# Attention values with rounded and low parts side by side as one stationary matrix

## The reference

```python
scores = q @ k.T / 8, causal; a = softmax(scores)
local = a @ v
q_p = phi(q)                       # where(x > 0, x, exp(x) - 1) + 1
mem_out = (q_p @ M_prev) / (q_p @ z_prev + 1e-06)
out = g * mem_out + (1 - g) * local     # g = sigmoid(beta), per head
x = out as [2304 tokens, 512]
x = elu(x @ w_in1) @ w_out1
x = (h * clip(h + 3, 0, 6) / 6) @ w_out2, h = x @ w_in2
```

## Time and profile before

| | us |
|---|---|
| median of 3 runs (1120.95 to 1123.28) | 1121.03 |
| the profiled execution | 1122.92 |
| its span | 1121.1 |
| PE busy (share of the span) | 1076.2 (96%) |
| DVE busy | 677.8 (60%) |
| ACT busy | 298.4 (27%) |
| POOL busy | 192.5 (17%) |

### The profile page before, as it was taken

One profiled execution on the slowest core, in us unless ns is written; L12 is line 12 of the kernel. 1 busy time (PEld: TensorE's weight loads), 2 busy tenths in 40 slices (PEclk: granted clock), 3 DMA queues, 4 the chain that ended last, 5 costly groups with the idle time before them and its releaser, 6 DMA issues.

```text
span 1121.1 us, 16386 instructions
## 1 busy us (share of the span) xinstructions
PE 1076.2 (96%) x6080; PEld 966.3 (86%) x6080; DVE 677.8 (60%) x1278; ACT 298.4 (27%) x737; POOL 192.5 (17%) x202
## 2 busy tenths in 40 slices
PE   5999999999889999999999999899999999999998
PEld 2667676676879999999999999898999999899997
DVE  5676766767388544545454468865656565565654
ACT  3666666666432212112121123301001010000100
POOL 3434434344265000000000025500000000000000
PEclk9999999999889999999999999999999999999999
DMA  4322121220134000000000014100000000000000
GB/s 162 119 97 101 52 101 56 98 101 20 38 113 132 1 1 1 0 0 0 0 0 0 0 37 131 57 1 13 15 0 28 0 28 0 0 28 0 28 0 28
DMA packets 16599, 44.56 MB, mean 40 GB/s; under 512 B 1968, under 2 KB 1968, under 8 KB 16560
## 3 DMA queue, kind: packets, MB, share of 16 engines
q1 hardware_dynamic: 16560, 44.05, 11.3%
HBM read 39.33 MB, written 4.72 MB: 39 GB/s over the span
## 4 chain that ended last, share of the span: by engine, by line
PE 89%; DVE 6%; issue 3%; ACT 1%; DMA 1%; SPq 0%; DVEq 0%
PE ps L473 35%; PE ps L494 18%; PE ps L486 17%; PE ps L450 8%; PE ps L384 3%; DVE pt_lo L751 2%; PE ps L379 1%; PE ps L459 1%; PE ps L428 1%; PE ps L418 1%; PE ps L387 1%; DVE x_all L795 1%; ACT r_rows L570 1%; PE ps L405 1%; DVE h_hi L824 1%
## 5 line engine op out<-in xcount | busy, mean ns | idle before, releaser
L473 PE MATMUL ps<-x_hi,w 128*128 128x384 f32 x1536 | 392.5, 336 | 0.0
L473 PEld LDWEIGHTS ps<-x_hi,w 128*128 128x128 f32 x1536 | 280.9, 189 | 7.4
L473 PE MATMUL ps<-x_lo,w 128*128 128x384 f32 x768 | 258.3, 336 | 0.0
L486 PE MATMUL ps<-h_hi,w 128*128 128x384 f32 x768 | 196.6, 336 | 6.0 <-DVE h_lo L826 6.0
L494 PE MATMUL ps<-w,h_hi 128*128 128x512 f32 x576 | 179.2, 392 | 3.1 <-DVE h_lo L826 3.1
L824 DVE CAST h_hi<-act_tmp 128x384 fp32r<-128x384 f32 x192 | 108.9, 567 | 100.9 <-PE ps L486 53.2
L486 PEld LDWEIGHTS ps<-h_hi,w 128*128 128x128 f32 x768 | 139.5, 189 | 7.0 <-DVE h_lo L826 7.0
L473 PEld LDWEIGHTS ps<-x_lo,w 128*128 128x128 f32 x768 | 144.7, 188 | 0.0
L296 POOL TENSOR_TENSOR w<-stage,w 128x1024 f32 (+1 forms) x32 | 77.7, 2436 | 358.3 <-ACT w L544 358.3
L486 PE MATMUL ps<-h_lo,w 128*128 128x384 f32 x384 | 129.0, 336 | 0.0
L494 PEld LDWEIGHTS ps<-w,h_hi 128*128 128x128 f32 x576 | 106.8, 188 | 22.1 <-issue 2.4
(11 more groups left out here) (110 smaller groups left out, 1233.8 us busy)
## 6 DMA issues: line engine op xcount, KB each, us to landing
nat<-nat_in SPq DMA_DIRECT2D x16, 768.0 KB, 5.4
qk<-qk_t SPq DMA_DIRECT2D x16, 608.0 KB, 3.8
stage<-w_in SPq DMA_DIRECT2D x32, 256.0 KB, 2.7
stage<-w_out SPq DMA_DIRECT2D x32, 256.0 KB, 2.9
out<-rows_out SPq DMA_DIRECT2D x18, 256.0 KB, 2.1
beta_sb<-beta SPq DMA_DIRECT2D x1, 4.0 KB, 6.5
```

Source lines behind the costliest of these rows:

```text
L473: mm = pe.matmul(ps[:, bank:bank + CHUNK], w[:, n, wp, 0, cols], xp[:, m, :], start=(m == 0 and part == 0), stop=(m == KM - 1 and part == 2))
L486: mm = pe.matmul(ps[:, Y_AT + 512 * m:Y_AT + 512 * m + CHUNK], w[:, n, wp, 1, cols], hp[:, n % 2, :], start=(n == 0 and part == 0), stop=( ...
```

## The change

V's rounded and low parts of one head stand side by side in one stationary matrix (`v_split`: 64 columns rounded, 64 low), and M's likewise (`m_split`). One pass with the rounded probabilities and one with the low ones replace three; the first 64 output partitions hold the rounded part's products, the other 64 those of the low part. (The product of both low parts is now added too.) Each head has an output bank of its own (banks 6 and 7) for rows 128 to 575. The rows 0 to 127 of both heads come in a piece of their own, `first_rows(p)`, behind `times_m(p)`, into a ring bank: the ring has a new place Q0 between G and C00. M's matmuls for rows 128 on take 64 rows of the array, one head each.

ScalarE's `low_rows(p)` copies the lower 64 partitions to SBUF at the head of slot 1, ahead of C00; VectorE's `sum_x(p)` adds them to the upper 64 in four pieces, in slot 1 behind the maximum and ahead of the row statistics; GpSimd's `store_x(p)` multiplies by the factors, between `phi_by_z(p+2)` and `split_vm(p+2)`.

```diff
+RING = (G, Q0, C00, C01, C10, C11, C2, C3, RMAIN, PHI, TAIL)
 # GpSimd
+            def store_x(p):
+                x = x_all[:, p * S:p * S + S]
+                pool.wait_ge(x_summed, p + 1)
+                pool.wait_ge(q0_summed, p + 1)
+                pool.wait_ge(r_done, p + 1)
+                pool.wait_ge(pt_hi_done, LOS * (p + 1))
+                pool.tensor_tensor(x, x, r_rows[:, :], ALU.mult).then_inc(x_stored, 1)
...
                     phi_by_z(p)
+                if p >= 2:
+                    store_x(p - 2)
+                if p < PAIRS:
                     split_vm(p)
 # TensorE: chunk_free
+                at = RING.index(c) - 2
+                before, q = RING[at], p if at >= 0 else p - 1
+                if before == Q0 and q >= 1:
+                    pe.wait_ge(q0_summed, q)
+                elif before == RMAIN and q >= 0:
+                    pe.wait_ge(r_done, q + 1)
+                elif before != Q0 and q >= 0:
+                    pe.wait_ge(pt_lo_done, LOS * q + LO_RANK[before] + 1)
 # times_v, times_m, first_rows
-                        pe.wait_ge(x_stored, p)
+                        pe.wait_ge(x_summed, p)
+                lo = max(P * t, P)
                 for a in range(2):
-                    for lo, hi in zip(cuts, cuts[1:]):
-                        for part, (v, pt) in enumerate(((v_hi, pt_hi), (v_lo, pt_hi), (v_hi, pt_lo))):
+                    for part, pt in enumerate((pt_hi, pt_lo)):
+                        mm = pe.matmul(ps[:, x_at(a) + lo - P:x_at(a) + S - P], v_tile(u, a, t), blocks(pt, a, t, lo, S),
+                                       start=(t == 0 and part == 0), stop=False)
...
+                for part, ph in enumerate((phi_t_hi, phi_t_lo)):
+                    for a in range(2):
+                        d = slice(D * a, D * a + D)
+                        mm = pe.matmul(ps[:, x_at(a):x_at(a) + S - P], m_tile(u, a)[d], ph[d, P:S], start=False, stop=(part == 1))
...
+            def first_rows(p):
+                u, at = p % 2, ring_at(p + 1, Q0)
+                chunk_free(p + 1, Q0)
+                for a in range(2):
+                    for part, pt in enumerate((pt_hi, pt_lo)):
+                        pe.matmul(ps[:, at + P * a:at + P * a + P], v_tile(u, a, 0), blocks(pt, a, 0, 0, P),
+                                  start=(a == 0 and part == 0), stop=False)
+                for part, ph in enumerate((phi_t_hi, phi_t_lo)):
+                    for a in range(2):
+                        mm = pe.matmul(ps[:, at + P * a:at + P * a + P], m_tile(u, a), ph[:, 0:P], start=False, stop=(a == 1 and part == 1))
+                mm.then_inc(q0_done, 1)
 # ScalarE
+            def low_rows(p):
+                if p >= 1:
+                    act.wait_ge(x_summed, p)
+                    act.wait_ge(q0_summed, p)
+                act.wait_ge(pv_done, 6 * (p + 1))
+                heads = ps[D:P, x_at(0):x_at(0) + 1024].rearrange("p (a q) -> p a q", a=2)
+                act.activation(x_low[D:P, :, P:S], heads[:, :, 0:S - P], ACT.Copy).then_inc(x_low_done, 1)
+                act.wait_ge(q0_done, p + 1)
+                at = ring_at(p + 1, Q0)
+                act.activation(x_low[D:P, :, 0:P], ps[D:P, at:at + 2 * P].rearrange("p (a q) -> p a q", a=2), ACT.Copy).then_inc(x_low_done, 1)
 # VectorE
+            def sum_x(p):
+                at, q0 = p * S, ring_at(p + 1, Q0)
+                dve.wait_ge(x_low_done, 2 * p + 1)
+                for a in range(2):
+                    add = dve.tensor_tensor(x_all[D * a:D * a + D, at + P:at + S], ps[0:D, x_at(a):x_at(a) + S - P], x_low[D:P, a, P:S], ALU.add)
+                add.then_inc(x_summed, 1)
+                dve.wait_ge(x_low_done, 2 * p + 2)
+                for a in range(2):
+                    add = dve.tensor_tensor(x_all[D * a:D * a + D, at:at + P], ps[0:D, q0 + P * a:q0 + P * a + P], x_low[D:P, a, 0:P], ALU.add)
+                add.then_inc(q0_summed, 1)
...
+                    if s == 1 and g >= 2:
+                        sum_x(g - 2)
                     if s == 1 and g >= 1:
                         row_stats(g - 1)
-                    if s == 1 and g >= 2:
-                        store_x(g - 2)
```

More of the change, by code:

```diff
@@ L105, in build @@
     phi = sb("phi", [2, QT, P])
[L106 to L109, removed]
+    v_split = sb("v_split", [2, QT, 2, 2, D], F32R)
+    m_split = sb("m_split", [2, 2, 2, D], F32R)
+    x_low = sb("x_low", [2, S])
     prob = sb("prob", [2, P_ALL])
@@ L150, in ring_at, with x_at @@
     def ring_at(p, c):
-        return 512 * (4 + (CHUNKS_OF * p + c) % 2)
-    X_AT = 7 * 512 - X_CUT
+        return 512 * (4 + (len(RING) * p + RING.index(c)) % 2)
+    def x_at(a):
+        return 512 * (6 + a)
     Y_AT = 4 * 512
@@ L178, in build @@
     pv_done = semaphore("pv_done")
+    q0_done = semaphore("q0_done")
+    x_low_done = semaphore("x_low_done")
+    x_summed = semaphore("x_summed")
+    q0_summed = semaphore("q0_summed")
     x_stored = semaphore("x_stored")
@@ L209, in build, with v_raw, v_tile, m_tile @@
     rows_sent = semaphore("rows_sent")
[L211 to L219, removed]
+    def v_raw(u):
+        return nat[:, u, 0:QT * P].rearrange("p (t a d) -> p t a d", t=QT, a=2)
+    def v_tile(u, a, t):
+        return v_split[:, u, t, a].rearrange("p h d -> p (h d)")
+    def m_tile(u, a):
+        return m_split[:, u, a].rearrange("p h d -> p (h d)")
     def rows_of(buf, i, a):
@@ L305, in split_vm @@
                 pool.wait_ge(nat_loaded[u], 16 * (p // 2 + 1))
-                if p == 0:
-                    pool.wait_ge(zeros_ready, 2)
                 if p >= 2:
[L309 to L312, removed]
+                    pool.wait_ge(q0_done, p - 1)
+                m_raw = nat[:, u, 2 * QT * P + P:NAT].rearrange("p (a d) -> p a d", a=2)
+                pool.tensor_scalar(m_split[:, u, :, 0], m_raw, 1.0, 1.0, ALU.mult, ALU.mult).then_inc(vm_rounded, 1)
+                pool.tensor_copy(v_split[:, u, :, :, 0], v_raw(u)).then_inc(vm_rounded, 1)
                 pool.wait_ge(vm_rounded, 2 * p + 2)
-                pool.tensor_tensor(m_lo[:, u, :], m_raw, m_hi.bitcast(F32)[:, u, :], ALU.subtract)
-                pool.tensor_tensor(v_placed(v_lo, u), v_all(nat, u), v_placed(v_hi.bitcast(F32), u), ALU.subtract).then_inc(vm_split, 1)
+                pool.tensor_tensor(m_split[:, u, :, 1], m_raw, m_split.bitcast(F32)[:, u, :, 0], ALU.subtract)
+                pool.tensor_tensor(v_split[:, u, :, :, 1], v_raw(u), v_split.bitcast(F32)[:, u, :, :, 0], ALU.subtract).then_inc(vm_split, 1)
+            def store_x(p):
[5 more added lines that the diff above has]
+                pool.tensor_tensor(x, x, r_rows[:, :], ALU.mult).then_inc(x_stored, 1)
             def phi_by_z(p):
@@ L358, in _ @@
             for n in range(APART, STAGES):
+                if n == EARLY:
+                    store_x(PAIRS - 1)
                 lo_weights(w[:, n], n, n)
@@ L413, in turn @@
                 elif c in (C2, C3):
-                    t = 2 + c - C2
+                    t = 2 if c == C2 else 3
                     for a in range(2):
@@ L510, in _ @@
                         times_m(g - 2)
+                        first_rows(g - 2)
                     if s == 2 and g >= 1:
@@ L521, in _ @@
             times_m(PAIRS - 1)
+            first_rows(PAIRS - 1)
             for n in range(KF):
@@ L549, in exp_rows @@
                 if s == 0 and p == 0:
-                    act.wait_ge(zeros_ready, 3)
+                    act.wait_ge(zeros_ready, 1)
                 if s == 0 and p >= 2:
@@ L577, in round_chunk @@
                     a, t = (c - C00) % 2, (c - C00) // 2
+                    if p >= 1 and c == C00:
+                        act.wait_ge(q0_done, p)
                     cp = act.activation(blocks(pt_hi, a, t, P * t, EDGE), ps[:, at:at + EDGE - P * t], ACT.Copy)
                 elif c in (C2, C3):
-                    t = 2 + c - C2
+                    t = 2 if c == C2 else 3
                     if c == C3 and p >= 1:
@@ L647, in _ @@
                 for s in range(QT):
+                    if s == 1 and g >= 2:
+                        low_rows(g - 2)
                     if g >= 1:
@@ L658, in _ @@
                         act.wait_ge(small_free, 1)
+                        act.wait_ge(x_stored, PAIRS - B + 1)
                         x_round(0, 0)
@@ L666, in _ @@
                         exp_tile(0, 0)
+            low_rows(PAIRS - 1)
             act.wait_ge(x_stored, PAIRS)
@@ L853, in _ @@
                         x_rest(0, 0)
-            store_x(PAIRS - 1)
+            sum_x(PAIRS - 1)
             for n in range(KF):
```

26 lines of the change are left out of this document (3 added, 23 removed).

## The result

| | before | after |
|---|---|---|
| median of 4 runs (lowest to highest) | 1122.03 us (1120.95 to 1123.28) | 1149.92 us (1148.77 to 1150.75) |
| ratio, 95% interval | | 1.0248 (1.0230 to 1.0265) |
| profiled execution: time, span, mean clock | 1122.92, 1121.1, 0.993 | 1150.63, 1148.4, 0.969 |

The forecast was 1153 us, from 1122 to 1166. The changed kernel is slower by 27.9 us.

A forecast was written before the change was run, and what follows sets the result against it. TensorE, busy 16.37 of 17.50 us per pair, looked like the bound, with relays through VectorE and ScalarE; 9 x 3.3 + 5 x 0.65 - 1.1 = +31.9 us on the 1121.03 median gave 1153 us, range 1122 to 1166.

The forecast's parts named there:

- TensorE ahead of the scores of slot 1, +0.32: TensorE's tile 4, M, first rows and switch back take 2.12 us against 1.80, so slot 1's scores start 0.32 later.
- rival 4: M's 64-row matmuls run one after another, adding 0.4 us ahead of the sums and 6 us to the total.
- The sums, 1.60: VectorE's four sums behind slot 1's maximum take 1.60 us, the middle of 1.44 overlapped and 1.76 end to end.
- C01's wait, idle time 2.7, key tile 0 later by 1.7, factors by 0.15: C01's transposes wait for the last sum: TensorE idle 2.7 us, key tile 0 1.7 later, factors 0.15 later.
- The saving behind it: Shorter TensorE work on key tiles 0 and 1, behind C01's wait, gives back 1.52 us per pair.
- Line 306 beside phi, 0.5: GpSimd's last queued operation moves beside VectorE's phi operations, one of which waits 0 to 0.73 us, taken as 0.5.
- A pair without a fall, +0.65: A steady attention pair at full clock grows by 0.65 us: 0.15 at the factors plus 0.5 at phi.
- Falls, 9 of 14 at +3.3: TensorE's new idle time drops the clock to 1.2 GHz in 9 of 14 pairs, each such pair 3.3 us longer.
- The total, +31.9: Whole kernel: 9 x 3.3 + 5 x 0.65 - 1.1 = +31.9 us, giving a median of 1153 us.
- Rival 1: The clock stays up and pairs cost 0.65 us, from 0.15 to 1.1: +2 to +14, centre 1129 us; chance 0.28.
- Group 1, -1.1: The first group with changed code has no sums before it and gains key tile 0's saving: -1.1 us.

The follow-up runs named there:

- experiment 9: Changed kernel with the four sums ordered by head, 448 and 128 columns of head 0, then of head 1: 1146.09 us in one run.
- experiment 1: Changed kernel with five unused f32 matmuls of 288 columns ahead of C01's transposes in groups 2 to 15, filling TensorE's idle time: 1142.20 us, ratio 1.0189.
- experiment 2: Changed kernel with VectorE summing the first rows before the two 448-column pieces, so C01 waits for the small sums only: 1145.30 us, ratio 1.0214.
- experiment 3: Changed kernel with VectorE's sums moved ahead of the maximum of slot 1: 1125.47 us, ratio 1.0036 to the kernel before.
- experiment 8: Changed kernel with only the row statistics moved ahead of the maximum, the sums still behind it: 1142.17 us, ratio 1.0183.
- experiment 5: Changed kernel with the sums ahead of the maximum and GpSimd's product at the head of its round: 1120.43 us, ratio 0.9991.
- experiment 6: Changed kernel with VectorE's slot 1 in the order row statistics, sums, maximum, low parts: 1108.01 us, ratio 0.9877 to the kernel before.
- experiment 4: Changed kernel with GpSimd's product of x and the factors moved to the head of its round: 1163.41 us, ratio 1.0377.

## Why the prediction held, and what it missed

- **TensorE ahead of the scores of slot 1, +0.32.** The scores of slot 1 begin 2.60 us after chunk G, before it was 2.19: +0.41. M's four 64-row matmuls take 0.60 (161.21 to 161.81) against 0.68 taken; rival 4 is out.
- **The sums, 1.60.** They take 1.89 (165.49 to 167.38), above the end-to-end bound of 1.76, since each takes a little more than taken and none overlaps the next. The middle was the wrong choice: the output changes its half of the partitions three times within the four, and experiment 9 shows that each change keeps an operation from overlapping the one before. The Trainium skill, page "VectorE: DVE Perf Modes", section "Two Vector instructions with no wait between them", had said so, and the trace agrees: by its rule the four sums came to 1.76, 0.16 above the term taken and nearer to what was measured.
- **C01's wait, idle time 2.7, key tile 0 later by 1.7, factors by 0.15.** Measured 2.77, then 2.08 (9.53 us after chunk G, before 7.45), then 0.62 (13.51 against 12.89). Of the missing 0.47 the sums and the start of the scores are 0.38. The saving behind it was 1.46, forecast 1.52.
- **Line 306 beside phi, 0.5.** Measured 0.47 (0.96 against 0.49) in pairs without a fall, and nothing in pairs with one, as said.
- **A pair without a fall, +0.65.** Measured +1.13, of which the two terms above make 1.09 (0.62 and 0.47). What was mis-sized is the relay.
- **Falls, 9 of 14 at +3.3.** The count was 10. The price was wrong: it was taken from the one fall of the trace before, 6.8 us long, and most falls here last 3.4, so a pair with one costs +1.94.
- **The total, +31.9.** The trace has 27.3. That these are so near is in part luck. The forecast put 23.9 on the falls (9 at 2.65 above a pair without) and 8.0 on the rest; filling the idle time (experiment 1) divides the measured 27.3 into 9.9 and 17.4. The mechanism was right, the falls were priced at more than twice and the rest at half of what they cost, and the two errors nearly cancelled. Rival 1, the same pairs with the clock up, was forecast at 1129 and came to 1142 in experiment 1. (The lower end of its sum is +1, not +2: 14 x 0.15 - 1.1.)
- **Group 1, -1.1.** It was -2.1. Key tile 0 gave 1.07 of it, as forecast (31.42 to 33.48 before, 30.60 to 31.59 after). Another 0.8 is the start of the clock and none of the change: the scores of slot 1 took 2.02 us before (25.55 to 27.57) and 1.21 after (25.64 to 26.85), against 1.06 in a steady pair, so the kernel before still ran at half speed there, though its profile gives the granted clock as 1.00.
- **Missed: GpSimd's relay.** The forecast moved the row statistics by 1.92 and looked only at the end of GpSimd's queue. Its middle, phi by z, feeds the norms. In the changed kernel this is late by 0.22 only, but it is next in line: it kept experiment 2 from its number and sets the pair of experiment 3.
- **Missed: the weights tile.** In group 3 GpSimd's queue ends with a split of 1024 columns (line 301, 2.37 us). Before, it ended ahead of phi (71.78 and 2.36, phi at 74.21); GpSimd's later statistics and its product bring it beside phi, which is blocked (the changed kernel in order of time):

```profile
75.19 2.37 POOL L301 TENSOR_TENSOR w<-stage,w 128x1024 fp32r<-128x1024 f32 x1
...
75.92 1.99 DVE L819 TENSOR_SCALAR phi<-nat 128x640 f32<-128x640 f32 x1 [2.00 <-PE ps L454]
```

  That is 1.5 us in one pair, and why experiments 1 to 3 all have a pair near 20.5. In experiment 8, where the statistics come first, the tile ends at 72.96, ahead of phi at 75.39, and group 3 takes no more than the other pairs with a fall (19.45). Where the sums stand ahead of the maximum (experiments 3, 5 and 6), group 3 is also longer because ScalarE splits weights there: 1.05 us ahead of the copy of the low shares in experiment 3 (58.43), so that C01 waits 1.45 instead of 0.51. All this was found in the traces; no run changed it alone.
- **What stays open.** The same 2.77 us of idle time brings a fall in 10 pairs of 14 here, in 8 of 14 in experiment 8 and in all 14 in experiment 4. No run was made to tell what decides it in the single pair.

## What to carry to other kernels

A resource that is freed later in another engine's order is a wait of its own: before adding a reader of a ring buffer, list what stands ahead of that reader on its engine, and put it ahead of anything that depends on the slot it holds back. Here the same arithmetic was 2.5% slower behind the maximum and 1.4% faster when spread ahead of and behind it. When an instruction is moved on an engine that feeds another, follow every reader of that other engine's queue, the middle too, and compare a reordered kernel with the old kernel reordered the same way, or the order's gain is credited to the change.

## What the runs showed of the hardware

- A fall of the granted clock to 1.2 GHz lasted 3.4 us in most cases (6.8 twice in the changed kernel's 14 pairs) and cost 1.33 us in a pair bound by relays (experiment 8). Four idle times of 0.25 to 0.88 us in each pair brought none in the steady pairs of experiment 3. Idle times of 2.77 us brought many, and so did 1.48 and 0.81 us with 1.7 us between them (experiment 2).
- Beside GpSimd on two SBUF inputs, VectorE's operation on two SBUF inputs waited until GpSimd's was done, small as it was: 20 columns took 1.36 us instead of 0.18 (experiment 4). Line 819 on 640 columns took 1.99 instead of 0.49. The Trainium skill, page "SBUF — State Buffer", section "Who interferes with whom", calls this an exclusive lock that blocks the later one wholly; the numbers agree. Two others were not held: VectorE's maximum, which reads PSUM, took its usual 1.23 with the product moved beside it (experiment 5), and line 827, a reduction of one SBUF input, took 0.82 beside it (171.69), as in the kernel before, which has no product on GpSimd.
- VectorE's sums on 64 partitions were not cheaper than operations on 128: 0.62 for 448 columns, against 0.55 for 128 partitions and 384 columns.
- Two 64-row matmuls of 448 columns on different halves of the rows ran beside each other, a pair every 0.31 us (161.21, 161.52). One after the other, at 0.20 each, they would take 0.40, so the gain was 1.3 times and not twice.
